# Windowed attention with two gated feed-forward layers: head units turned one slot later, zero products moved, first front product begun one step later

## Chip, cores and metric

One NeuronCore of a Trainium2 chip. The metric is the device time of one execution in microseconds (us), median of the runs of a kernel.

## What is computed

Attention of 2 batches x 8 heads, 768 positions, head size 64, with 4 sink keys and a window of 128; its output, as 1536 tokens of 512 features, goes through a SiLU-gated layer and a leaky-ReLU layer:

```python
scores = np.where(is_sink | in_window, scale * q @ k.T, -1e9)
a = exp(scores - max) / (sum + 1e-9);  attn = a @ v
x = attn.transpose(0, 2, 1, 3).reshape(1536, 512)
y = (silu(x @ w_gate) * (x @ w_val)) @ w_out          # d_ff 1536
h = y @ w_in2
out = (max(h, 0) + alpha * min(h, 0)) @ w_out2        # d_ff 2048
```

## The kernel before, in words

**Units and slots.** The attention is cut into 48 units: one tile of 128 queries for one pair of heads. One unit passes through seven steps on five engines: PE makes the scores (`scores`, L1833 to L1841), DVE masks them and takes the maximum (`take`, `maximum`), ACT takes exponentials and sums (`exps`), DVE inverts the sums (`invert`, L2286), POOL multiplies by the inverses (`normalise`, L1780), PE turns (transposes) the result (`turn`, L1861), DVE copies it out of PSUM under the window's triangles (`spread`, L2297), and PE multiplies by V (`values`, L1886; in the head with a product for the sinks, L1896). A list, `plan`, is written out ahead of time and every engine walks through it in order. Its item `slot` holds four unit numbers: scores of w; exponentials, inversion and normalising of w-1; turn of w-2; values of w-3 (`LAG = 3`).

**The head.** The first 16 units (`early`) are worked "pair by pair" with nothing else for PE to do: slots w = 0 to 18, which have indices 0 to 18. In a head slot PE does scores, then turn, then values. For units with sinks ACT copies the turned sink columns (`copy_sinks`, L2091) behind the exponentials of the slot; the product L1896 waits for that copy. The p tiles alternate between two PSUM halves, so scores of unit w wait for the exponentials of w-2. `keep_busy` (L2054) multiplies zeros, to keep PE occupied: 6 products at the start, 6 before scores of unit 2, and 2, 1, 1 and 2 before the turns of units 0, 1, 2 and 14. The first front product of the feed-forward layer ("begin") stands behind slot 16. In each head slot POOL also splits half a piece of weights into a high and a low part (`split_piece`, L1698 and L1699).

**The main part.** The other 32 units are spread over the products of the first layer ("front" and "back" chunks, L1932 and L2047), one slot every 4 us or so: w = 16 to 50, indices 19 to 53. There PE does scores, then values, then turn, then front or back products. POOL does, in this order, normalise of unit w-1 and then the jobs given to the slot (`in_slot`): two jobs in slots of even index, one in those of odd index, or one where sums (`tsum`) follow. A job is a whole piece of weights, or a sum. The pieces are numbered r in the order of the jobs; 0 to 5 are split in the head, 6 is the first of the main part. There are 4 buffers for raw pieces, so piece r can be loaded once piece r-4 has been split.

**The loads.** SP issues every load from one queue, in order, and waits on semaphores in between:

```python
for n in range(early, len(slot_plan) + 1):
    if n_pairs * c - 5 <= n and c < n_quads:
        load_values(c)      # waits: values of units < 4*(c-2)
        c += 1
    if n_pairs * c - 8 <= n and n % n_pairs == 0 and c < n_quads and c > RING + 1:
        load_keys(c)        # waits: scores of units < 4*(c-2)
    while r < len(raws) and slot_of_raw(r) <= n:
        load_piece(r)       # waits: piece r-4 split
        r += 1
```

`slot_of_raw(r)` is the index of the slot that holds the job that frees the buffer of piece r. So n counts slot indices, and the loads of keys and values (c is a group of four units) stand at fixed indices in the queue. Sorted by this loop the queue reads, before: v6, p10, k7, p11, p12, p13, p14, p15, v7, p16, k8, p17 and so on (k is keys and queries, v values, p a raw piece).

Of the kernel before, what the change touches and what calls it, by code (L numbers as in the profile page):

```python
# [804 lines left out]
def build_windowed(nc, qt, kt, vt, vs, pieces, alpha_t, out, n_batch, n_sink, ff_b, ff_c, scale):  # L805
# [7 lines left out]
    early = quads_t * n_pairs  # L813
# [61 lines left out]
    LAG = 3  # L875

    def slot(w, lo, hi):
        return ("slot", tuple(u if lo <= u < hi else None for u in range(w, w - LAG - 1, -1)))

    def fronts(g):  # L880

        return [("front", (g, f, part, half)) for part in range(parts[g[0]] - 1) for f in range(F) for half in range(2)]
# [24 lines left out]
    def emit_slot(item):  # L907
        plan.append(item)
        done = item[1][3]
        if done is not None and done % n_pairs == n_pairs - 1:  # L910
            c = done // n_pairs
            plan.append(("x", c))
            return [("x_rest", c)]
        return []
# [42 lines left out]
    first_g = groups_b[0]  # L957
    begun = {(first_g, 0, 0): n_k - 1}
    late_rest = []
    for w in range(early + LAG):  # L960
        item = slot(w, 0, early)
        rest = emit_slot(item)
        plan.extend(late_rest)
        late_rest = rest
        if w == early:
            plan.append(("begin", (first_g, 0, 0, 0)))
        if (item[1][3] or 0) == early - 1:
            plan.extend(rest)
# [161 lines left out]
    for what, key in chunks:  # L1130
        home = None
        if what == "back":
            g, t, d = key
            if g[0] == "B" and t != single:
                home = (rest_of_b if g != pair_b[-1] else (2, 3, 4, 0, 1, 2, 3, 4))[4 * (t - 1) + d]
            elif g[0] == "C" and (t != single or g[1] > 2):
                had["all"] = had.get("all", -1) + 1
                home = had["all"] % 3
            elif g == groups_c[2]:
                home = d % 2  # L1140
        elif what == "strip" or key[3] == 1 or (key[0][0] == "C" and key[0][1] > 2):
            continue
        if home is None:

            home = in_turn[(len(front_home) + len(back_home)) % 4]
# [143 lines left out]
    slot_plan = [n for n, (what, _) in enumerate(plan) if what == "slot"]  # L1289
    in_slot = [[] for _ in slot_plan]  # L1290

    def ready_at(job):
        what, key = job
        name = ("piece", key) if what == "piece" else ("sums", (key[0], key[1], key[2] // 2))
        return plan_at[cell_ahead[name]] if name in cell_ahead else -1

    next_job = first_pieces
    for n in range(early + LAG, len(slot_plan)):
        for _ in range(1 if n % 2 or plan[slot_plan[n] + 1][0] == "tsum" else 2):
            if next_job < len(jobs) and ready_at(jobs[next_job]) < slot_plan[n]:  # L1300
                in_slot[n].append(jobs[next_job])
                next_job += 1
# [3 lines left out]
    n = next(n for n, job in enumerate(late_jobs) if ready_at(job) >= turn_at)  # L1306
# [4 lines left out]
    with ctx:  # L1311
# [95 lines left out]
        att_ps = ctx.enter_context(nc.psum_tensor("att_ps", [P, 4 * BANK], F32))  # L1407
        ffn_ps = ctx.enter_context(nc.psum_tensor("ffn_ps", [P, 4 * BANK], F32))

        def bank(ps, n):  # L1410
            return ps[:, n * BANK:(n + 1) * BANK]

        def home(n, last):

            return ffn_ps if n < last and n % 2 else att_ps
# [10 lines left out]
        def before(n, last):  # L1426

            return n - 2 if n <= last else n - 1
# [115 lines left out]
        def head_sinks(u):  # L1544

            return u < early and has_prev(place(u)[0])

        def head_sinks_until(u):
            return sum(head_sinks(v) for v in range(u + 1))
# [103 lines left out]
        def _(pool):  # L1653
# [75 lines left out]
            def pair_sum(stage, n, m):  # L1729

                name = T_ORDER[stage][n]
                if stage == "B":
                    at = (slice(None), slice(None), block_cols(m))
                    if name == "T1":
                        pool.wait_ge(xcopy_done, 2 * m + 2)
                        pool.wait_ge(xlo_done, quads_t + 2 * m + 1)
                    elif name == "T2":
                        pool.wait_ge(xlo_done, quads_t + 2 * m + 2)
                else:
                    at = (slice(None), m, slice(None))  # L1740
                    if name == "T1":
                        pool.wait_ge(x2lo_done, x2_no[pair[0], m])
                        pool.wait_ge(evac_done, evac_no[pair_b[-1], pair[1], m])
                    elif name == "T2":
                        pool.wait_ge(evac_done, evac_no[pair_b[-1], pair[1], half_k + m])
                    elif name == "T4":
                        pool.wait_ge(x2lo_done, x2_no[pair[0], half_k + m])
                if n:
                    pool.wait_ge(tsum_done, tsum_no[stage, n - 1, m])
                q11, q21, q12, q22 = (q[at] for q in quarters[stage])  # L1750
                t1, t2 = (sum_sb(stage, T_ORDER[stage].index(t))[at] for t in ("T1", "T2"))
                a, b = {"T1": (q12, q11), "T2": (q22, t1), "T3": (q22, q12), "T4": (q21, t2)}[name]
                pool.tensor_tensor(sum_sb(stage, n)[at], a, b, ALU.subtract).then_inc(tsum_done, 1)
# [39 lines left out]
            n_slot = -1  # L1793
            for what, units in plan:
                if what == "tsum":
                    pair_sum(*units)
                if what != "slot":
                    continue
                n_slot += 1
                if units[1] is not None:  # L1800
                    normalise(units[1])
                if n_slot < early + LAG:
                    if n_slot in (early - 4, early - 3, early, early + 1):
                        split_v_sink(sinks_split // 2, sinks_split % 2)
                        sinks_split += 1
                    elif halves_split < 2 * first_pieces:
                        split_piece(jobs[halves_split // 2][1], 2, halves_split % 2)
                        halves_split += 1
                else:
                    for job in in_slot[n_slot]:  # L1810
                        do(job)
# [4 lines left out]
        def _(pe):  # L1816
# [24 lines left out]
                        last = pe.matmul(ps[:, 0:2 * cols], q, both, start=True, stop=True)  # L1841
                    last.then_inc(scores_done[h], 1)

            fills = {0: 2, 1: 1, 2: 1, early - 2: 2}

            def turn(u):
                s, n = divmod(u, n_pairs)
                if u == 0:
                    pe.wait_ge(pool_own, own["consts"])
                ahead = before(u, early)  # L1850
                if ahead >= 0:
                    pe.wait_ge(pt_done, ahead + 1)
                    if head_sinks(ahead):
                        pe.wait_ge(head_sink_done, head_sinks_until(ahead))
                    elif ahead % n_pairs == n_pairs - 1 and stacked_sinks(ahead // n_pairs):
                        pe.wait_ge(sink_done, sinks_until(ahead // n_pairs))
                if u in fills:
                    keep_busy(fills[u], bank(home(u, early), 2))
                pe.wait_ge(norm_done, u + 1)
                for h in range(2):  # L1860
                    last = pe.transpose(turn_ps(u)[:, block_cols(h)], p_sb[:, u % 8, h * (cols + n_sink):h * (cols + n_sink) + P], ident[:, :])  # L1861
                if head_sinks(u):
                    last = pe.transpose(turn_ps(u)[0:2 * n_sink, block_cols(2)], p_sb[:, u % 8, P:P + 2 * n_sink], ident[:, :])
                elif n == n_pairs - 1 and stacked_sinks(s):
                    pe.wait_ge(gathered, sinks_until(s))
                    last = pe.transpose(turn_ps(u)[0:stacked, block_cols(2)], p_sink[:, s % 2, :], ident[:, :])
                last.then_inc(turned, 1)
# [183 lines left out]
            def keep_busy(n, ps):  # L2051

                for _ in range(n):
                    pe.matmul(ps, h_hi[:, 0, 0:P], h_hi[:, 0, :], start=True, stop=True, skip_group_check=True)  # L2054
# [3 lines left out]
            for what, n in plan:  # L2058
                if what == "front":
                    front(*n)  # L2060
                elif what == "back":
                    back(*n)
                elif what == "strip":
                    strip(*n)
                elif what == "begin":
                    begin_front(*n)
                elif what == "slot":
                    if n[0] == 2:
                        keep_busy(6, bank(att_ps, 2))
                    if n[0] is not None:  # L2070
                        scores(n[0])
                    if n[2] is not None and n[2] < early:

                        turn(n[2])
                        if n[3] is not None:
                            values(n[3])
                    else:
                        if n[3] is not None:
                            values(n[3])
                        if n[2] is not None:  # L2080
                            turn(n[2])
# [452 lines left out]
```

## Time and profile before

| | us |
|---|---|
| median of 3 runs | 635.02 (634.78 to 650.35) |
| profiled execution, its own time | 635.71 |
| its span, first to last instruction | 634.0 |
| granted TensorE clock | 1.000 |

Times in the rows are microseconds from the start of the span; 1.7 us of the profiled execution lie around the span. "idle before" with a name is the time that the engine stood still ahead of an instruction, and what released it. PE's records overlap, since products are pipelined: the distance from start to start is what one costs.

### The profile page before, as it was taken

What the parts mean: (1) busy time and instruction counts of PE and PEld (TensorE: products, weight loads), DVE (VectorE), ACT (ScalarE), POOL (GpSimd) and SP (SyncE); (2) the same over time, 40 slices, a digit from 0 to 9 for tenths busy, and PEclk for the clock granted to TensorE, in tenths of its full rate; (3) what the DMA queues carried; (4) which work ended last, traced back from release to release, by engine and by line L of the source; (5) the groups of instructions that cost most, each with busy time, mean ns of one, the idle gap of its engine ahead of it and who ended that gap; (6) DMA issues with size and microseconds to landing.
All of it is one profiled execution on the core that took longest, in us unless ns stands there. A gap on an engine that the chain in (4) does not pass through costs nothing.

```text
span 634.0 us, 9482 instructions
## 1 busy us (share of the span) xinstructions
PE 624.4 (98%) x3113; PEld 488.7 (77%) x3113; DVE 410.7 (65%) x689; ACT 245.5 (39%) x597; POOL 452.7 (71%) x597
## 2 busy tenths in 40 slices
PE   8899999999999999999999999999999999999997
PEld 5557776777777888888887888887888888888886
DVE  4855476575476866565647474898686567756474
ACT  4646545536435542121212121445534324442150
POOL 6857778787788999998989664689999987810000
PEclk9999999999999999999999999999999999999999
DMA  9064333421213111121102322100222212000004
GB/s 309 19 189 146 98 104 117 134 68 52 66 68 100 34 34 39 66 87 42 68 34 66 98 70 66 33 18 18 67 67 67 68 66 84 18 0 1 0 18 182
DMA packets 34016, 45.69 MB, mean 72 GB/s; under 512 B 2888, under 2 KB 15176, under 8 KB 33968
## 3 DMA queue, kind: packets, MB, share of 16 engines
q1 hardware_dynamic: 33824, 44.83, 21.7%
q8 instruction: 25, 0.41, 0.3%
q10 hardware_dynamic: 144, 0.26, 0.2%
q14 instruction: 23, 0.19, 0.1%
HBM read 41.93 MB, written 3.15 MB: 71 GB/s over the span
## 4 chain that ended last, share of the span: by engine, by line
PE 93%; ACT 1%; DMA 1%; DVE 1%; POOL 1%; issue 1%; SPq 0%; DVEq 0%; ACTq 0%; POOLq 0%
PE ffn_ps L2047 29%; PE att_ps L2022 24%; PE ffn_ps L1932 14%; PE att_ps L2047 8%; PE ffn_ps L2022 7%; PE att_ps L1886 3%; PE att_ps L1841 3%; PE att_ps L1861 2%; PE att_ps L1932 1%; DMA raw_weights<-pieces 1%; POOL scratch L1780 1%; PE att_ps L1903 1%; DMA k_sb<-kt 1%; PE ffn_ps L1886 1%; ACT scratch L2104 1%
## 5 line engine op out<-in xcount | busy, mean ns | idle before, releaser
L1699 POOL TENSOR_TENSOR w_lo<-raw_weights,w_hi 128x512 fp32r<-128x512 f32 (+1 forms) x128 | 155.4, 1214 | 10.3
L1698 POOL CAST w_hi<-raw_weights 128x512 fp32r<-128x512 f32 (+1 forms) x128 | 80.9, 632 | 33.5 <-PE ffn_ps L2047 17.2
L2409 DVE TENSOR_TENSOR scratch<-ffn_ps,scratch 128x512 f32<-128x512 f32 x108 | 74.1, 687 | 34.8 <-PE ffn_ps L2047 34.2
L1727 POOL TENSOR_TENSOR w_lo<-part_sum,w_hi 128x256 fp32r<-128x256 f32 x80 | 59.7, 747 | 6.4
L1932 PE MATMUL ffn_ps<-x_hi,w_hi 128*128 128x512 f32 x152 | 61.9, 407 | 0.1
L1932 PE MATMUL ffn_ps<-x_hi,w_lo 128*128 128x512 f32 x152 | 59.4, 391 | 0.0
L1932 PE MATMUL ffn_ps<-x_lo,w_hi 128*128 128x512 f32 x152 | 59.3, 390 | 0.0
L1780 POOL TENSOR_TENSOR scratch<-scratch,inv 128x264 f32<-128x264 f32 (+1 forms) x48 | 30.4, 634 | 31.5 <-DVE inv L2286 31.3
L2047 PE MATMUL ffn_ps<-h_hi,w_hi 128*128 128x512 f32 x130 | 51.6, 397 | 0.0
L2047 PE MATMUL ffn_ps<-h_hi,w_lo 128*128 128x512 f32 x130 | 50.7, 390 | 0.0
L2047 PE MATMUL ffn_ps<-h_lo,w_hi 128*128 128x512 f32 x130 | 50.6, 389 | 0.0
L2193 ACT ACTIVATE value_sb<-att_ps 128x512 f32<-128x512 f32 x14 | 8.4, 599 | 94.2 <-PE att_ps L2022 94.2
L2022 PE MATMUL att_ps<-t_hi,w_hi 128*128 128x512 f32 x112 | 44.2, 394 | 0.0
L2022 PE MATMUL att_ps<-t_hi,w_lo 128*128 128x512 f32 x112 | 44.0, 393 | 0.0
L2022 PE MATMUL att_ps<-t_lo,w_hi 128*128 128x512 f32 x112 | 43.7, 390 | 0.0
L2022 PE MATMUL att_ps<-x_hi,w_hi 128*128 128x512 f32 x108 | 42.8, 396 | 0.0
L2022 PE MATMUL att_ps<-x_hi,w_lo 128*128 128x512 f32 x108 | 42.4, 393 | 0.0
L2022 PE MATMUL att_ps<-x_lo,w_hi 128*128 128x512 f32 x108 | 42.1, 390 | 0.0
L2269 DVE COPY_PREDICATED att_ps<-take_prev,att_ps 128x256 f32<-128x256 int32 x36 | 15.3, 426 | 39.5 <-PE att_ps L1841 28.7
L1726 POOL CAST w_hi<-part_sum 128x256 fp32r<-128x256 f32 x80 | 35.8, 447 | 5.1
L2097 ACT ACTIVATE bias<-top 128x2 f32<-128x2 f32 x48 | 9.7, 202 | 72.0 <-DVE top L2281 72.0
L2182 ACT ACTIVATE gate_sb<-gate_sb,minus_alpha 128x512 f32<-128x512 f32 x48 | 34.8, 725 | 1.6
(213 smaller groups left out, 1586.0 us busy)
## 6 DMA issues: line engine op xcount, KB each, us to landing
raw_weights<-pieces SPq DMA_DIRECT2D x122, 256.0 KB, 2.7
k_sb<-kt SPq DMA_DIRECT2D x12, 264.0 KB, 3.5
v_sb<-vt SPq DMA_DIRECT2D x12, 256.0 KB, 3.6
out<-scratch SPq DMA_DIRECT2D x12, 256.0 KB, 2.0
q_sb<-qt SPq DMA_DIRECT2D x11, 256.0 KB, 4.2
scratch<-vs SPq DMA_DIRECT2D x1, 384.0 KB, 7.0
q_sb<-qt ACTq DMA_DIRECT2D x1, 256.0 KB, 3.5
scratch<-vs SPq DMA_DIRECT2D x1, 16.0 KB
```

Of the source, the lines that this page charges most:

```text
L1698: chain(pool.tensor_copy(hi, raw[:, r % n_raw, at]))
L1699: last = pool.tensor_tensor(lo, raw[:, r % n_raw, at], hi.bitcast(F32), ALU.subtract)
L1726: chain(pool.tensor_copy(hi, s))
L1727: pool.tensor_tensor(lo, s, hi.bitcast(F32), ALU.subtract).then_inc(split_done, 1)
L1780: pool.tensor_tensor(rows, rows, inv[:, u % 4, :].unsqueeze(2).to_broadcast([P, 2, cols - at]), ALU.mult).then_inc(norm_done, 1)
L1841: last = pe.matmul(ps[:, 0:2 * cols], q, both, start=True, stop=True)
L1886: last = pe.matmul(x[d, :], v_sb[:, g, ring, d], pt_sb[:, u % 2, m, h, :], start=n == 0 and m == 0, stop=not has_prev(c), skip_group_check ...
L1932: last = pe.matmul(ps, w_parts[a][:, block_cols(kk)], x_parts(kk)[b], start=kk == 0 and (a, b) == (0, 0), stop=kk == n_k - 1 and (a, b) == ...
L2022: last = pe.matmul(ps, w_parts[a][:, block_cols(at * half_k + kk)], b_parts[b][:, kk, :], start=first and kk == 0 and (a, b) == (0, 0), st ...
L2047: last = pe.matmul(ps, lhs, rhs, start=f == 0 and (a, b) == (0, 0), stop=f == F - 1 and (a, b) == (1, 0))
L2182: act.activation(gate_of(h), gate_of(h), ACT.Copy, scale=minus_alpha[:, col:col + 1]).then_inc(relu_done, 1)
L2409: ins = dve.tensor_tensor(to, back_ps(key), total, ALU.add)
```

## The change

Head slots hold other units: scores of w, exponentials to normalising of w-1, turn of w-3 (was w-2), values of w-4 (was w-3). So the head has 20 slots, w = 0 to 19. "begin" stands behind slot 18, which holds the turn of unit 15; before it stood behind the slot with the turn of unit 14. The zero products are now 6 before scores of unit 2 and 4 before scores of unit 3, beside the 6 at the start; those before the turns are gone. The start of POOL's jobs and the end of its head work go by the new length. SP's loop is not touched.

```diff
+    HEAD_LAG = 4
+
+    def head_slot(w):
+
+        return ("slot", tuple(u if 0 <= u < early else None for u in (w, w - 1, w - HEAD_LAG + 1, w - HEAD_LAG)))
...
-    for w in range(early + LAG):
-        item = slot(w, 0, early)
+    for w in range(early + HEAD_LAG):
+        item = head_slot(w)
         rest = emit_slot(item)
         plan.extend(late_rest)
         late_rest = rest
-        if w == early:
+        if w == early + 2:
             plan.append(("begin", (first_g, 0, 0, 0)))
...
     next_job = first_pieces
-    for n in range(early + LAG, len(slot_plan)):
+    for n in range(early + HEAD_LAG, len(slot_plan)):
         for _ in range(1 if n % 2 or plan[slot_plan[n] + 1][0] == "tsum" else 2):
...
-                if n_slot < early + LAG:
+                if n_slot < early + HEAD_LAG:
                     if n_slot in (early - 4, early - 3, early, early + 1):
...
-            fills = {0: 2, 1: 1, 2: 1, early - 2: 2}
+            fills = {2: 6, 3: 4}
...
-                if u in fills:
-                    keep_busy(fills[u], bank(home(u, early), 2))
                 pe.wait_ge(norm_done, u + 1)
...
                 elif what == "slot":
-                    if n[0] == 2:
-                        keep_busy(6, bank(att_ps, 2))
+                    if n[0] in fills:
+                        keep_busy(fills[n[0]], bank(att_ps, 2))
```

## Rows read from the trace of the kernel before

**Rows 1.** The page: busy time of PE, share of the span, instructions.

```profile
PE 624.4 (98%) x3113; PEld 488.7 (77%) x3113; DVE 410.7 (65%) x689; ACT 245.5 (39%) x597; POOL 452.7 (71%) x597
```

**Rows 2.** Waits of the whole span: in total, times, longest.

```profile
POOL w_hi L1698 <- DMA raw_weights<-pieces: 8.5, 6, 3.0
...
PE ffn_ps L1861 <- POOL scratch L1780: 3.4, 6, 0.8
```

**Rows 3.** Busy time by engine in head slots 8 to 11.

```profile
20.75:29.39 8.64, 7.47 (x70) 4.20 (x68) 6.99 (x19) 5.57 (x29) 6.88 (x13) 1.00 0.01 4
```

**Rows 4.** Timeline of PE in the head: start, duration, instruction, idle before.

```profile
1.52 2.93 PE L2054 MATMUL att_ps<-h_hi 128*128 128x512 f32 x6 [1.52 <-DVE h_hi L2441]
4.51 1.25 PE L1841 MATMUL att_ps<-k_sb,q_sb 64*128 64x264 f32 x4
...
22.83 0.72 PE L1841 MATMUL ffn_ps<-k_sb,q_sb 64*128 64x264 f32 x4
24.02 0.41 PE L1861 MATMUL ffn_ps<-ident,scratch 128*128 128x128 f32 x2 [0.48 <-POOL scratch L1780]
...
25.31 0.72 PE L1841 MATMUL att_ps<-k_sb,q_sb 64*128 64x264 f32 x4
...
35.44 0.49 PE L1833 MATMUL ffn_ps<-k_sb,q_sb 64*128 64x128 f32 x4
...
42.09 0.44 PE L1886 MATMUL ffn_ps<-scratch,v_sb 128*64 128x128 f32 x4
```

**Rows 5.** Timeline of ACT in head slot 15: the copy of sink columns.

```profile
38.85 0.25 ACT L2091 ACTIVATE scratch<-ffn_ps 8x128 f32<-8x128 f32 x1
```

**Rows 6.** Timeline of SP's queue: the issues of keys 7 to 11.

```profile
55.76 0.55 SPq L1598 DMA_DIRECT2D k_sb<-kt  x1
...
75.10 0.55 SPq L1598 DMA_DIRECT2D k_sb<-kt  x1
...
93.58 0.55 SPq L1598 DMA_DIRECT2D k_sb<-kt  x1
...
112.26 0.56 SPq L1598 DMA_DIRECT2D k_sb<-kt  x1
...
131.93 0.56 SPq L1598 DMA_DIRECT2D k_sb<-kt  x1
```

**Rows 7.** Timeline of POOL: pieces that waited for their load, and the normalising behind them.

```profile
60.78 0.61 POOL L1698 CAST w_hi<-raw_weights 128x512 fp32r<-128x512 f32 x1 [0.94 <-DMA raw_weights<-pieces]
...
62.72 1.07 POOL L1780 TENSOR_TENSOR scratch<-scratch,inv 128x264 f32<-128x264 f32 x1
...
118.92 0.61 POOL L1698 CAST w_hi<-raw_weights 128x512 fp32r<-128x512 f32 x1 [2.98 <-DMA raw_weights<-pieces]
...
120.84 0.63 POOL L1780 TENSOR_TENSOR scratch<-scratch,inv 128x264 f32<-128x264 f32 x1
```

**Rows 8.** Timeline of PE, main part: scores of unit 19 (54.91), turn of 18 (60.50), and so on.

```profile
54.91 0.50 PE L1835 MATMUL att_ps<-k_sb,q_sb 64*128 64x132 f32 x4 [0.43 <-ACT scratch L2104]
...
60.50 0.44 PE L1861 MATMUL att_ps<-ident,scratch 128*128 128x128 f32 x2
...
74.28 0.72 PE L1841 MATMUL att_ps<-k_sb,q_sb 64*128 64x264 f32 x4
...
79.64 0.44 PE L1861 MATMUL att_ps<-ident,scratch 128*128 128x128 f32 x2
...
92.97 0.49 PE L1833 MATMUL att_ps<-k_sb,q_sb 64*128 64x128 f32 x4
...
98.67 0.44 PE L1861 MATMUL att_ps<-ident,scratch 128*128 128x128 f32 x2
...
121.62 0.41 PE L1861 MATMUL att_ps<-ident,scratch 128*128 128x128 f32 x2 [0.19 <-POOL scratch L1780]
...
131.07 0.50 PE L1835 MATMUL att_ps<-k_sb,q_sb 64*128 64x132 f32 x4
...
136.67 0.44 PE L1861 MATMUL att_ps<-ident,scratch 128*128 128x128 f32 x2
```

## The prediction

> **What bounds the kernel now.** The page first: PE is busy for 624.4 of 634.0 us [rows 1]. So only 9.6 us of the span are free of PE work, and a change can win little but lose as much as it likes: every wait that it puts in front of PE is added to the end. Next the list of waits by engine: PE waited 3.4 us in six pieces for POOL's normalising, and all six stand in the head [rows 2]. The table of stretches shows a group of four head slots: 8.64 us long, PE busy for 7.47, and DVE and POOL at 6.99 and 6.88, not far behind [rows 3]. The timeline of PE shows where it comes from: scores of unit 9 start at 22.83, the turn in the same slot only at 24.02, after 0.48 us of idle [rows 4]. Outside the head PE hardly waits, and so what the head gains reaches the end, if nothing behind it gets worse. That was my second reading: POOL waited 8.5 us in six pieces for loads of weights [rows 2]. Today this costs PE 0.19 us, once [rows 8], since it ends just in time. The change moves POOL's jobs and leaves SP's queue where it is, so I followed that queue item by item.
>
> **The head, gain.** With the turn at w-3 the normalised unit is a whole slot older when PE comes to it. In a group of four slots it is done 1.3 us or more ahead (normalising 0.6 us, slots of about 1.9), so the 3.4 us of waits go. Of the zero products, six go and four come (two before the turn of 14 are a further 0.5 us on the path; those before turns 0 to 2 and the four new ones stand where PE waits for exponentials of the first units, and cost about nothing). That is 3.9 us at most.
>
> What is late next is ACT's copy of the sink columns. It stands last in ACT's slot, behind the exponentials: in slot 15 scores start at 35.44 and the copy ends at 38.85 + 0.25 = 39.10, 3.66 us later [rows 4, 5]. The product of the next slot needs it, before and after the change alike, but the slots get shorter. Slots with tile 0 cost PE about 1.2 us and the next ones 2.1, together 3.3, where the copy with the product behind it asks for 3.6: 0.3 us three times, 0.9. After slot 15 PE arrives 2.6 us behind the scores (1.5 for the slot, 0.45 for a turn, 0.6 for values) at a copy that ends 3.7 behind them: 1.1 us. Gain of the head: 3.9 - 0.9 - 1.1 = **1.9, taken as 2.0 us**; bounds 0.5 (DVE and POOL, near full, delay more) and 3.9. The first front product moved behind the last turn is the same product at another place in the order: it is work that covers the wait for the values of unit 15, which end at 42.5 today [rows 4], and I cost it at nothing (if the cover is missing, 0.3 us).
>
> **The main part, loss.** The head has one more slot, so each slot of the main part has an index higher by one. POOL's first job moves with it (index 20), but the choice of two jobs for even indices now falls on the other slots of w, and SP's loads of keys and values stand at the old indices, one slot early in w. SP's queue then reads v6, k7, p10, p11, p12, p13, p14, v7, p15, k8, p16 instead of v6, p10, k7, p11 and so on: one piece fewer ahead of each barrier. What the barrier waits for is unchanged: keys 7 wait for the scores of unit 19, keys 8 for those of 23, keys 9 of 27, keys 11 of 35. POOL needs more by then: in the slot w=18 it has pieces 9 and 10 to split, and behind them in its queue stands the normalising of unit 18, which PE turns in slot w=20. But piece 10 is now behind keys 7, and they go out only with the scores of unit 19. So POOL stands still over a whole slot, and behind it the normalising, and behind that PE's turn with all front products.
>
> The price follows from rows that show the same chain one slot later. Scores of 19 at 54.91, keys 7 issued at 55.76 (0.85 later) [rows 6, 8]; the piece behind them lands and POOL starts at 60.78 (5.02 later) [rows 7]; the piece takes 62.72 - 60.78 = 1.94; normalising to turn takes 121.62 - 120.84 = 0.78 [rows 7, 8]. Together 8.59 us behind the scores of 19. PE wants the turn of 18 at 60.50, 5.59 behind them [rows 8]. **Stall 3.0 us.** The same at the other barriers, with scores, issue and turn from [rows 6, 8]:
> - keys 8, piece 16, turn of 22: 0.82 + 5.02 + 1.94 + 0.78 = 8.56, wanted at 79.64 - 74.28 = 5.36: 3.2 us.
> - keys 9, piece 22, turn of 26: 8.35, wanted at 98.67 - 92.97 = 5.70: 2.65 us.
> - keys 10: the sums behind slots 27 and 28 take a job away from each, and the two orders meet again; piece 28 waits for its load (2.98 us) and the turn of 31 for 0.19, as now. No change.
> - keys 11, piece 33 (now the second job of w=34), turn of 34: 8.60, wanted at 136.67 - 131.07 = 5.60: 3.0 us.
>
> Sum 3.0 + 3.2 + 2.65 + 3.0 = **11.9 us**. The barrier of keys 10 shows that the load can take 6.66 instead of 5.02 (112.26 to 118.92) [rows 6, 7]; with that at all four the sum is 11.9 + 4 x 1.64 = 18.5. I take 5.02, since it stands at keys 7 itself and the queue behind keys 11 is short. Behind slot 34 the jobs are sums, which need no load, and further on pieces are far ahead of their users: nothing more. Values 7 and on hold back one piece as well (15, 21), but that one lands before the piece behind the keys and so ends inside the same stall.
>
> Sum: 635.7 (the profiled execution, whose span is 634.0) - 2.0 + 11.9 = 645.6; the median of the runs is 0.7 lower, so **644.9 us**, 1.6% slower.
>
> **The clock.** TensorE's granted clock is 1.00 in the stretch of the head that I read [rows 3]. But six zero products at the start take 2.93 us and four scores at 4.51 take 1.25, against 0.72 for four of the same form at 22.83 [rows 4]: the engine runs at 1.2 GHz for its first 4 us of work and at 2.4 after them. That stretch cost some 2 us. So if a stall of 3 us throws it back to the low level, each costs 2 us more. No idle stretch of that length after the start is in this trace. The Trainium skill (TensorE: Matmul & The Clock Gate, Why this matters for your kernels) asks for no long idle gaps between bursts of products, or the clock halves; by it each stall forecast here would be priced as in the rival of the falling clock below. What it says of keeping the engine busy at the start speaks against taking zero products out of the first slots too.
>
> **Rivals.**
> - *The queue doesn't bite*, since a load lands sooner than I think or POOL's order leaves room: only the head's gain, 635.0 - 2.0 = 633.0 (631 to 634.5). For it: POOL had 0.9 to 3 us of such waits already and PE paid 0.19. Against: 8.6 against 5.6 us is a clear gap; even a load that lands 2 us sooner leaves a stall of 1 us. Chance 0.14.
> - *It bites in part*, with one or two of the four stalls hidden: 636 to 641. Chance 0.09.
> - *The clock falls* in the stalls: four times 2 us more, 652.9, slower by more than 2%; it decides at a stall of 3 us between the units, and from two falls on the time is past 648. Chance 0.12.
> - *Loads take 6.66 us* at most barriers, with many pieces queued behind one another: 644.9 + up to 6.6, 648 to 651.5. Chance 0.13.
> - The forecast, 641 to 648: chance 0.52.
>
> **Range and chances.** A measurement of this kernel tells about 2% from no change, 12.7 us. Leaving out the first rival below and a tail above, the range is 636 to 653. Slower by over 2% is past 647.7: 0.12 + 0.13 + 0.01 = 0.26. Faster by over 2% would need more than all of PE's idle time: 0.01. Within: 0.73.
>
> **What the profile after would show.** PE's waits for L1780 in the head gone, and groups of four head slots at 7.4 to 7.9 us; waits of PE's turn (L1861) for POOL's normalising of 2.6 to 3.3 us each, at about 58, 81, 103 and 144 us, some 12 us in total; POOL's idle time before L1698 up from 8.5 to over 20 us with the load as releaser; in SP's queue keys 7 ahead of any piece. PE's product of the front at one spacing on both sides of a stall, if the clock holds. Wrong would be: head waits that move to ACT's copy by more than 2 us, or waits of PE that are missing in the main part, which would mean that the loads are not what holds POOL.

## Result and the profile after

The changed kernel takes **656.10 us** (median of 4 runs, 655.83 to 657.79), the kernel before 635.03 (median of 4): a ratio of **1.0339 [1.0317, 1.036]**, 3.4% slower. The forecast was 644.9 with a range to 653, so the time lies 3.1 us above the range. A run of the kernel before that took 650.35 us, and others like it, are left out of every ratio here, though a median takes in all runs unless it says otherwise. The profiled execution took 656.12 us, its span is 654.4 (634.0 before), the granted clock 0.984 (1.000 before).

The page of the changed kernel: busy time of PE, then its busy share and its granted clock in 40 slices of 16.4 us each. Against [rows 1] PE is busy for 8.4 us more, though it does two instructions fewer.

```profile
PE 632.8 (97%) x3111; PEld 494.6 (76%) x3111; DVE 405.0 (62%) x689; ACT 246.2 (38%) x597; POOL 451.3 (69%) x597
...
PE   8997977998999999999999999999999999999998
PEclk9998989997999999999999999999999999999999
```

In the busy row PE is below 90% in slices 1, 4, 6, 7, 10 and 40 (a 9 stands for 90% or more), and the granted clock is below 90% in slices 4, 6 and 10. The kernel before has an 8 in slices 1 and 2 and a 7 in slice 40, 9 in all others, and nothing but 9 in its clock. So there are two losses in the same part of the kernel: time in which PE stands still, and time in which it works at a lower clock. The second sits inside "busy", and the list of waits doesn't show it.

Waits of the changed kernel, whole span (lines are shifted by 4 to 6: L1704 is L1698 of before, L1786 is L1780, L1865 is L1861), to be put beside [rows 2]:

```profile
POOL w_hi L1704 <- DMA raw_weights<-pieces: 35.8, 12, 6.4
...
PE att_ps L1865 <- POOL scratch L1786: 14.2, 4, 4.1
```

The 3.4 us of PE's waits in the head are gone. In their place stand four waits of 14.2 us together, and POOL's waits for loads have gone from 8.5 to 35.8 us. The timeline of PE shows the four, and the head ahead of them:

```profile
19.01 0.72 PE L1847 MATMUL att_ps<-k_sb,q_sb 64*128 64x264 f32 x4
...
26.98 0.72 PE L1847 MATMUL att_ps<-k_sb,q_sb 64*128 64x264 f32 x4
...
35.75 0.66 PE L1890 MATMUL ffn_ps<-scratch,v_sb 128*64 128x128 f32 x8 [0.51 <-DVE scratch L2301]
...
42.49 0.50 PE L1841 MATMUL att_ps<-k_sb,q_sb 64*128 64x132 f32 x4
...
53.35 0.50 PE L1841 MATMUL att_ps<-k_sb,q_sb 64*128 64x132 f32 x4 [0.43 <-ACT scratch L2108]
...
62.65 0.66 PE L1865 MATMUL att_ps<-ident,scratch 128*128 128x128 f32 x2 [3.64 <-POOL scratch L1786]
62.96 0.78 PE L1936 MATMUL ffn_ps<-x_hi,w_hi 128*128 128x512 f32 x1
...
68.17 0.40 PE L1936 MATMUL ffn_ps<-x_hi,w_hi 128*128 128x512 f32 x1
68.40 0.40 PE L1936 MATMUL ffn_ps<-x_lo,w_hi 128*128 128x512 f32 x1
...
88.51 0.62 PE L1865 MATMUL att_ps<-ident,scratch 128*128 128x128 f32 x2 [4.12 <-POOL scratch L1786]
...
112.30 0.52 PE L1865 MATMUL att_ps<-ident,scratch 128*128 128x128 f32 x2 [3.38 <-POOL scratch L1786]
...
154.71 0.66 PE L1865 MATMUL att_ps<-ident,scratch 128*128 128x128 f32 x2 [3.01 <-POOL scratch L1786]
```

Scores of unit 19 start at 53.35, the turn of unit 18 at 62.65 instead of some 3.6 us sooner. Behind it 12 products take 68.17 - 62.96 = 5.21 us from start to start, 0.43 each; then they go on at 0.23. What holds the turn is seen in SP's queue, beside [rows 6]:

```profile
43.76 0.58 SPq L1611 DMA_DIRECT2D v_sb<-vt  x1
54.20 0.54 SPq L1604 DMA_DIRECT2D k_sb<-kt  x1
...
55.47 6.81 SPq L1616 DMA_DIRECT2D raw_weights<-pieces  x5
```

and in POOL's timeline, beside [rows 7]:

```profile
59.97 0.61 POOL L1704 CAST w_hi<-raw_weights 128x512 fp32r<-128x512 f32 x1 [6.43 <-DMA raw_weights<-pieces]
...
61.88 0.63 POOL L1786 TENSOR_TENSOR scratch<-scratch,inv 128x264 f32<-128x264 f32 x1
...
85.83 0.61 POOL L1704 CAST w_hi<-raw_weights 128x512 fp32r<-128x512 f32 x1 [4.55 <-DMA raw_weights<-pieces]
...
109.63 0.61 POOL L1704 CAST w_hi<-raw_weights 128x512 fp32r<-128x512 f32 x1 [3.67 <-DMA raw_weights<-pieces]
...
152.03 0.61 POOL L1704 CAST w_hi<-raw_weights 128x512 fp32r<-128x512 f32 x1 [3.49 <-DMA raw_weights<-pieces]
```

Read as one chain: no piece is issued between values 6 (43.76) and keys 7 (54.20, 0.85 behind the scores that they wait for); the first piece behind the keys lets POOL start at 59.97; POOL takes 1.91 for it; the normalising at 61.88 is followed 0.77 later by PE's turn. It is the chain of the prediction, link by link.

**Where the 20.4 us of span went.** The scores of unit 16 start at 42.49; before they started at 44.05, so the head gives 1.56 back. The stalls add 3.64 + 4.12 + 3.38 + 3.01 = 14.15, and the 0.19 of before [rows 8] is gone: +13.96. What is left is 20.4 + 1.56 - 13.96 = **8.0 us**, to which no wait belongs. The table of stretches shows what it is (columns: stretch, its length, busy time and instructions of PE, PEld, DVE, ACT, POOL, then the granted clock, DMA share, GB/s):

```profile
60.00:64.00 4.00, 1.35 (x5) 1.19 (x6) 0.65 (x2) 0.81 (x5) 3.84 (x5) 0.66 0.50 155
64.00:66.00 2.00, 2.00 (x6) 1.62 (x5) 0.96 (x2) 0.00 (x0) 1.94 (x4) 0.50 0.03 12
66.00:68.00 2.00, 2.00 (x6) 1.52 (x6) 0.00 (x0) 0.00 (x0) 1.92 (x3) 0.50 0.00 0
68.00:70.00 2.00, 2.00 (x12) 1.38 (x10) 0.00 (x0) 0.00 (x0) 1.55 (x2) 0.98 0.00 0
...
90.00:92.00 2.00, 2.00 (x6) 1.52 (x6) 1.69 (x3) 0.00 (x0) 1.94 (x4) 0.51 0.00 0
...
114.00:116.00 2.00, 2.00 (x7) 1.57 (x6) 1.13 (x2) 0.00 (x0) 1.92 (x4) 0.53 0.00 0
...
156.00:158.00 2.00, 2.00 (x6) 1.59 (x5) 0.10 (x1) 0.00 (x0) 1.92 (x4) 0.50 0.00 0
```

From 64 to 68 PE is busy all the time and does 6 instructions in 2 us where it does 12 from 68 on: the clock is at 0.50, the level of 1.2 GHz. It came down in the stall and is back at 68. The last three rows show the same behind the other three stalls. A full PE row with a low instruction count beside it is the sign to look for.

The distances of the products give the price a second time. Behind the first stall it is 12 x (0.43 - 0.23) = 2.4 us. Behind the others PE's timeline has 7, 8 and 11 products at 0.43 before they go on at 0.23, some 1.5, 1.6 and 2.3 us more, and together 7.8 (an estimate from these distances).

### The profile page after: what moved, and what is told of

Its sections match the earlier page's. It is cut to its first block, busy times and chain, and to the rows that moved or that the text cites. A ratio compares the mean times of both kernels' runs of the same rounds, so it can differ in the third digit from the quotient of the medians.

```text
span 654.4 us, 9479 instructions
## 1 busy us (share of the span) xinstructions
PE 632.8 (97%) x3111; PEld 494.6 (76%) x3111; DVE 405.0 (62%) x689; ACT 246.2 (38%) x597; POOL 451.3 (69%) x597
## 4 chain that ended last, share of the span: by engine, by line
PE 89%; DMA 5%; POOL 2%; ACT 2%; DVE 1%; issue 1%; SPq 0%; DVEq 0%; POOLq 0%; ACTq 0%
PE ffn_ps L2051 27%; PE att_ps L2026 23%; PE ffn_ps L1936 14%; PE att_ps L2051 7%; PE ffn_ps L2026 6%; DMA raw_weights<-pieces 4%; PE att_ps L1890 3%; PE att_ps L1847 2%; PE att_ps L1865 2%; POOL w_lo L1705 1%; PE att_ps L1936 1%; ACT scratch L2108 1%; POOL w_hi L1704 1%; DMA k_sb<-kt 1%; PE ffn_ps L1847 0%
## 5 line engine op out<-in xcount | busy, mean ns | idle before, releaser
L1704 POOL CAST w_hi<-raw_weights 128x512 fp32r<-128x512 f32 (+1 forms) x128 | 78.9, 617 | 62.0 <-DMA raw_weights<-pieces 35.8
L1936 PE MATMUL ffn_ps<-x_hi,w_hi 128*128 128x512 f32 x152 | 64.5, 424 | 0.1
L1936 PE MATMUL ffn_ps<-x_hi,w_lo 128*128 128x512 f32 x152 | 61.7, 406 | 0.0
L1936 PE MATMUL ffn_ps<-x_lo,w_hi 128*128 128x512 f32 x152 | 61.6, 406 | 0.0
L1786 POOL TENSOR_TENSOR scratch<-scratch,inv 128x264 f32<-128x264 f32 (+1 forms) x48 | 30.7, 639 | 26.2 <-DVE inv L2290 26.0
L2186 ACT ACTIVATE gate_sb<-gate_sb,minus_alpha 128x512 f32<-128x512 f32 x48 | 34.8, 725 | 1.6
```

Source lines behind the costliest of these rows:

```text
L1704: chain(pool.tensor_copy(hi, raw[:, r % n_raw, at]))
L1786: pool.tensor_tensor(rows, rows, inv[:, u % 4, :].unsqueeze(2).to_broadcast([P, 2, cols - at]), ALU.mult).then_inc(norm_done, 1)
L1936: last = pe.matmul(ps, w_parts[a][:, block_cols(kk)], x_parts(kk)[b], start=kk == 0 and (a, b) == (0, 0), stop=kk == n_k - 1 and (a, b) == ...
L2186: act.activation(gate_of(h), gate_of(h), ACT.Copy, scale=minus_alpha[:, col:col + 1]).then_inc(relu_done, 1)
```

## Experiments

The theory after the result: SP's loads of keys and values stand one slot too early against POOL's jobs, PE stalls four times for that, and each stall lowers the clock behind it. The rivals: the new head itself costs the time; the choice of two jobs in even slots does; the 8 us are something other than the clock. "Before" is always the kernel before, run on the same chip beside the experiment. The changed kernel itself was not run again beside them; it has 656.10 against 635.03 for the kernel before, which took 635.45 to 635.53 beside the experiments.

### The queue moved along by one slot

In the changed kernel SP's two conditions take n - 1, so that keys and values stand in the same slots of w as before. The jobs stay as the change has them.

```diff
-                if n_pairs * c - 5 <= n and c < n_quads:
+                if n_pairs * c - 5 <= n - 1 and c < n_quads:
...
-                if n_pairs * c - 8 <= n and n % n_pairs == 0 and c < n_quads and c > RING + 1:
+                if n_pairs * c - 8 <= n - 1 and (n - 1) % n_pairs == 0 and c < n_quads and c > RING + 1:
```

> The changed kernel with one edit: SP's conditions for keys and values count from the longer head (n - 1 in place of n). Theory (the stalls come from keys and values that stand one slot too early in SP's queue): the pieces 10, 16, 22 and 33 are again ahead of their barrier, the four waits of PE for the normalising (14.2 us) go, with them the stretches at half clock; only the head's gain is left: 633.5 us, 22.6 less than the changed kernel. Rival (the order of the jobs, two in other slots, holds POOL by itself): waits of PE of several us stay, 640 to 656. Rival (the head itself costs): waits gone and the time still over 636.

Measured: 633.52 us (633.10 to 633.59), before 635.45, ratio 0.9967 [0.9955, 0.998]. SP's queue of this kernel now has two pieces between values 6 and keys 7:

```profile
44.13 0.58 SPq L1611 DMA_DIRECT2D v_sb<-vt  x1
44.76 1.80 SPq L1616 DMA_DIRECT2D raw_weights<-pieces  x2
54.56 0.55 SPq L1604 DMA_DIRECT2D k_sb<-kt  x1
```

Its waits: POOL waits 9.9 us for loads in place of 35.8, near to [rows 2], and PE's turn waits for the normalising 0.2 us in place of 14.2.

```profile
POOL w_hi L1704 <- DMA raw_weights<-pieces: 9.9, 7, 2.3
```

So two conditions in a queue that the change did not touch are worth 656.10 - 633.52 = 22.6 us, and what is left of the change is a gain of a third of a per cent. The whole loss hangs on the numbering.

### The queue and the jobs moved along

The same, and the choice of one or two jobs goes by n - 1 too.

```diff
-        for _ in range(1 if n % 2 or plan[slot_plan[n] + 1][0] == "tsum" else 2):
+        for _ in range(1 if (n - 1) % 2 or plan[slot_plan[n] + 1][0] == "tsum" else 2):
```

> The changed kernel with SP's conditions and the choice of slots with two jobs both counted from the longer head, so that the main part is that of before, in the order of its units. Theory: 633.4 us, waits of PE for normalising in the main part 0.2 us in all as before; the difference to before, 1.6 us, is the head alone. Rival (the head's gain is lost again on the way): 635.

Measured: 633.30 us (632.90 to 634.50), ratio 0.9968 [0.9958, 0.9978]. It can't be told from the kernel above; with the queue right, no cost shows for the place of the second job. In its trace no turn in the main part waits for the normalising.

### Only the jobs moved along

The last edit alone, SP's queue as in the change.

> The changed kernel with one edit: the slots that get two jobs are again those of before in the order of the units (n - 1 in place of n); SP's queue stays as the change left it. Theory (the stall needs both, a load one slot too early in the queue and a second job ahead of the normalising): with one job in the slots w=18, 22 and 26 the normalising gets through, the stalls of 3 to 4 us go; where a slot with two jobs now meets late loads (w=31, and the sums behind piece 33) 0.5 to 2 us each may stay: 634 to 637 us, clock 1.00. Rival (the queue alone makes the loss): 650 to 656.

Measured: 644.69 us (640.51 to 647.04), before 635.53, ratio 1.0132 [1.0098, 1.0166]. This missed: it is 7.7 us above the upper end expected. I had followed keys only. Its timelines show the stalls at the barriers of values (a barrier is a load in the queue that waits, with everything behind it). The first of them, SP:

```profile
69.17 0.55 SPq L1611 DMA_DIRECT2D v_sb<-vt  x1
69.76 1.20 SPq L1616 DMA_DIRECT2D raw_weights<-pieces  x2
```

POOL and PE, whose turn waits behind it:

```profile
73.04 0.61 POOL L1704 CAST w_hi<-raw_weights 128x512 fp32r<-128x512 f32 x1 [3.99 <-DMA raw_weights<-pieces]
...
74.95 0.62 POOL L1786 TENSOR_TENSOR scratch<-scratch,inv 128x264 f32<-128x264 f32 x1
```

```profile
75.72 0.41 PE L1865 MATMUL att_ps<-ident,scratch 128*128 128x128 f32 x2 [1.83 <-POOL scratch L1786]
```

The piece for the second job of slot w=21 is freed one slot later than in the change and so falls behind values 7, which wait for the values of unit 19. PE waits four times, 7.3 us in all and at most 2.3 at a time. In the profiled run (640.51) the clock held at 1.000; the other three had 0.992 to 0.995 and took 644.3 to 647.0. So the jobs alone take off half of the loss and do not heal the change; a queue one slot too early costs with either choice of jobs, through values with one and through keys with the other.

### The old head with the queue one slot too early

The kernel before, its head, zero products and "begin" untouched; SP's conditions and the choice of jobs take n + 1 instead of n (and SP's loop starts one index sooner). This is the loss of the change without any other part of it.

```diff
-        for _ in range(1 if n % 2 or plan[slot_plan[n] + 1][0] == "tsum" else 2):
+        for _ in range(1 if (n + 1) % 2 or plan[slot_plan[n] + 1][0] == "tsum" else 2):
...
-            for n in range(early, len(slot_plan) + 1):
-                if n_pairs * c - 5 <= n and c < n_quads:
+            for n in range(early - 1, len(slot_plan) + 1):
+                if n_pairs * c - 5 <= n + 1 and c < n_quads:
...
-                if n_pairs * c - 8 <= n and n % n_pairs == 0 and c < n_quads and c > RING + 1:
+                if n_pairs * c - 8 <= n + 1 and (n + 1) % n_pairs == 0 and c < n_quads and c > RING + 1:
```

> The kernel before, its head untouched, with only the indices of the main part taken one higher for SP's keys and values and for the slots with two jobs. Theory: this alone makes the loss: 635.0 + 14.0 of stalls + 8 of half clock = 657 us, four waits of PE for the normalising of units 18, 22, 26 and 34. Rival (the stalls need the new head, for example since SP's first loads come earlier): 635 to 645.

Measured: 657.60 us as the median of three runs (654.87 to 657.93; a fourth, of 670.96 at a clock of 0.957, is left out), ratio 1.0336 [1.0312, 1.0359]. Its waits show those of the old head (3.2, as in [rows 2]) and the stalls of the changed kernel side by side (14.9 in five pieces, of which 14.2 in four lie between 58 and 160 us):

```profile
PE att_ps L1861 <- POOL scratch L1780: 14.9, 5, 4.2
...
PE ffn_ps L1861 <- POOL scratch L1780: 3.2, 6, 0.8
```

The new head is not where the loss comes from.

### The stalls filled with products

In the changed kernel PE does 13 products of 512 columns with real data ahead of the turns of units 18, 22, 26 and 34. They write into the bank that the turn then overwrites, so the result is unchanged. 13 x 0.23 = 3.0 us is nearly the stall: the stall stays, but PE isn't idle in it.

```diff
+                if u in (18, 22, 26, 34):
+                    for _ in range(13):
+                        pe.matmul(bank(att_ps, 2), x_hi[:, 0, 0:P], x_hi[:, 0, :], start=True, stop=True, skip_group_check=True)
                 pe.wait_ge(norm_done, u + 1)
```

> The changed kernel with 13 products of real data, written to the bank of the turn and overwritten by it, ahead of PE's wait for the normalising of units 18, 22, 26 and 34. They take 13 x 0.23 = 3.0 us, inside the stalls of 3.0 to 4.1. Theory (the stalls themselves cost 14 us and a fall of the granted clock behind them 8 us): the stalls stay as gaps of 1 us or less beside the products, the clock stays at 2.4 GHz, 648 us. Rival (the rest of the loss has another cause than the clock): 656.

Measured: 647.46 us (647.10 to 648.37), ratio 1.0193 [1.0178, 1.0209], granted clock 1.000 in all four runs. Its timeline of PE at the first stall:

```profile
58.90 3.26 PE L1865 MATMUL att_ps<-x_hi 128*128 128x512 f32 x13
62.48 0.44 PE L1868 MATMUL att_ps<-ident,scratch 128*128 128x128 f32 x2 [0.31 <-POOL scratch L1786]
62.67 0.48 PE L1939 MATMUL ffn_ps<-x_hi,w_hi 128*128 128x512 f32 x1
...
65.49 0.39 PE L1939 MATMUL ffn_ps<-x_hi,w_hi 128*128 128x512 f32 x1
```

The turn comes at 62.48 (62.65 in the changed kernel): the same stall. The 12 products behind it take 65.49 - 62.67 = 2.82 us instead of 5.21, so 2.4 us of clock at this stall. POOL's wait for loads is unchanged, 34.8 in 12 pieces. The kernel does more work and is 656.10 - 647.46 = **8.6 us faster** (by the two ratios, 1.0339 and 1.0193, it would be 9.3); that is the price of the clock, and it is near the 8.0 us left over above.

### The stalls half filled

The same with 6 products, which leaves 1.6 to 2.6 us of idle time at each.

> The changed kernel with 6 products of real data instead of 13 ahead of the four awaited turns. They cover 1.4 us of each stall and leave gaps of 1.6 to 2.5 us. Theory (only the long gaps let the clock fall): clock 1.00 and the time of the run with 13 products, 647.5, since the stalls end by the load and not by PE. Rival (gaps of 2 us are enough): a part of the 8 us comes back, 650 to 655.

Measured: 650.99 us, ratio 1.0253 [1.0205, 1.0301], but from 648.18 to 657.52 over four runs, with clocks of 0.997, 0.989, 0.997 and 0.995. Two of the four stalls in the profiled run, in PE's timeline:

```profile
84.68 0.69 PE L1868 MATMUL att_ps<-ident,scratch 128*128 128x128 f32 x2 [2.09 <-POOL scratch L1786]
...
150.71 0.44 PE L1868 MATMUL att_ps<-ident,scratch 128*128 128x128 f32 x2 [2.63 <-POOL scratch L1786]
```

and the stretches around them:

```profile
80.00:88.00 8.00, 5.91 (x27) 4.43 (x28) 4.28 (x9) 1.85 (x7) 5.68 (x8) 0.79 0.44 157
...
150.00:158.00 8.00, 7.29 (x41) 5.52 (x42) 2.79 (x7) 2.22 (x7) 7.49 (x14) 1.00 0.00 0
```

The clock fell behind an idle time of 2.09 us and did not behind those of 1.6, 2.06 and 2.63. So the expectation, a clock of 1.00 and 647.5, missed. At this length the outcome differs from place to place, and the mean clock from run to run; the length of the gap alone doesn't decide it. What does is left open. The clock isn't the whole spread either: 0.997 against 0.989 of some 650 us is about 5 us (an estimate), and the two runs lie 657.52 - 648.18 = 9.3 us apart.

### The zero products alone

The kernel before with 6 zero products before scores of unit 2 and 4 before those of unit 3, and none before turns. Those of unit 3 write to the other half of PSUM than in the changed kernel.

```diff
-            fills = {0: 2, 1: 1, 2: 1, early - 2: 2}
+            fills = {2: 6, 3: 4}
...
-                if u in fills:
-                    keep_busy(fills[u], bank(home(u, early), 2))
...
-                    if n[0] == 2:
-                        keep_busy(6, bank(att_ps, 2))
+                    if n[0] in fills:
+                        keep_busy(fills[n[0]], bank(att_ps if n[0] == 2 else ffn_ps, 2))
```

> The kernel before with only its zero products changed as in the change (none before the turns, 4 before scores of unit 3, these in the other half of PSUM), units turned as before. Theory (zero products stand where PE waits anyway): 635.0, within 0.5 of before. Rival (they are a part of the gain): 633.5 to 634.3; rival (they keep the clock up in the first slots): slower by 1 us or more, a clock under 1.00.

Measured: 635.04 us over 12 runs, before 635.53 (19 runs), ratio 0.999 [0.9978, 1.0002]: no difference that can be told, though the interval leaves room for a gain of up to 1.4 us (0.22% of 635). Nine runs took 634.34 to 636.47 at a clock of 1.000, three took 647.40 to 649.55 at 0.968 to 0.973. No trace of one of the three was kept.

### The first front product at its old place

The kernel with queue and jobs moved along, with "begin" behind slot 16 again.

```diff
-        if w == early + 2:
+        if w == early:
```

(The edits of the queue and the jobs are as above.)

> The kernel with SP's conditions and the jobs counted from the longer head, but the first front product begun behind slot 16 as before the change, in place of behind the last turn. Theory (the product is the same work at another place): 633.3 as with it, within 0.3. Rival (behind the last turn it covers the wait for the values of unit 15): slower by 0.4 to 0.7 us, 633.9.

Measured: 633.38 us against 633.30, ratio 0.9962 [0.9948, 0.9977]. The place of "begin" is worth nothing that can be told, as forecast. What is left for the gain of 2 us is the later turn, with whatever the zero products give: at most 1.4 us by the interval above, and in the trace of that run the scores of unit 16 start at 43.55 in place of 44.05. The later turn was not run without them, so how the gain is split is not shown.

### Without the four zero products before unit 3

The kernel with queue and jobs moved along, with `fills = {2: 6}`.

> The kernel with SP's conditions and the jobs counted from the longer head, without the 4 zero products before scores of unit 3. They take 0.9 us in the profile of the changed kernel, ahead of scores that are ready at about 9.1 us there. Theory: up to 0.4 us less, 632.9 to 633.3, clock 1.00 all through. Rival (they keep the clock up in the sparse first slots): a granted clock under 1.00 in the first 20 us and 634 to 636.

Measured: median 633.57 us, ratio 0.998 [0.9957, 1.0003], but the 12 runs fall into two groups: eight from 632.62 to 633.78 at a clock of at least 0.999, four at 637.48, 640.23, 640.24 and 643.81 at 0.979 to 0.989. The profiled run is one of the four. Its stretches in the head:

```profile
12.00:16.00 4.00, 2.91 (x21) 1.71 (x23) 3.40 (x9) 3.01 (x17) 3.83 (x7) 0.80 1.05 313
16.00:20.00 4.00, 4.00 (x21) 2.19 (x23) 1.52 (x4) 2.13 (x12) 2.95 (x6) 0.50 0.23 82
20.00:24.00 4.00, 4.00 (x24) 2.15 (x21) 1.38 (x5) 1.22 (x6) 1.70 (x3) 0.50 0.00 0
24.00:30.00 6.00, 6.00 (x40) 3.12 (x39) 4.23 (x12) 3.29 (x15) 3.37 (x6) 0.66 0.02 4
```

Two of these stretches in the kernel with the four products:

```profile
12.00:16.00 4.00, 3.76 (x36) 2.21 (x37) 3.76 (x10) 3.02 (x16) 2.50 (x5) 1.00 1.06 290
...
20.00:24.00 4.00, 3.60 (x34) 2.04 (x34) 3.23 (x9) 3.05 (x14) 3.84 (x8) 1.00 0.02 6
```

In the first, PE stands still for 1.44 us ahead of the scores at 13.09; then the clock falls to 0.50 and stays there for over 8 us, though PE is busy all the time. But the two runs differ before the first of the four products would have come. The six zero products before scores of unit 2, which both kernels have, in the run without the four and then in the run with them:

```profile
6.71 2.93 PE L2058 MATMUL att_ps<-h_hi 128*128 128x512 f32 x6
```

```profile
6.65 1.64 PE L2058 MATMUL att_ps<-h_hi 128*128 128x512 f32 x6
```

So the slow products of the start lasted longer in the run without the four (its scores at 9.57 still took 1.25 us), and what is missing behind them can't be the reason for that part. (The granted clock is given as 1.00 for these first microseconds in both; the lower level is read from the durations.) The other eight runs of the same kernel kept a clock of at least 0.999 without the four products.

The rival on record, that the four keep the clock up, was priced at 634 to 636; four runs of 12 went that way and took 4 to 11 us more than the other eight. None of the 27 runs of the four kernels that have the new head with all zero products and a queue in time had a clock below 0.999, which speaks for the four products as a guard. Against it, the old head with all ten products (the run with the zero products alone) had three of 12 runs at 0.968 to 0.973. That the four products prevent the fall is therefore suggested and not shown; when nothing falls, leaving them out gains nothing that can be told.

### The queue two slots later still

The changed kernel with the jobs moved along and SP's conditions at n - 3, and so with more pieces ahead of each barrier than the kernel before has.

> The kernel with the jobs counted from the longer head and SP's conditions two slots later still (n - 3), so that more pieces stand ahead of each barrier of keys and values. Theory: POOL's waits for loads in the main part (5 us and more in the kernel with n - 1) shrink to 1 us or less, the waits of PE for the normalising (0.2 to 0.9 us) go: 632.5 to 633.2. Rival (keys or values then come late for PE): waits of PE for loads, over 634.

Measured: 633.34 us (633.14 to 635.11), before 635.48, ratio 0.9967 [0.9954, 0.998]. POOL waits for loads 6.3 us in 4 pieces (12.8 in 7 with the queue and the jobs moved along by one). The expectation was 1 us or less and 632.5 to 633.2, so the waits missed and the time lies 0.1 above. Half of POOL's waits went and the time stayed the same as with n - 1 (633.30): what POOL still waits for is hidden.

## Why the prediction was wrong

**The mechanism held.** SP's queue one slot too early, four stalls of the turn behind the normalising behind a piece behind the keys: forecast to begin at about 58, 81, 103 and 144 us, the waits began at 59.01, 84.39, 108.92 and 151.70 (the starts of the turns, 62.65, 88.51, 112.30 and 154.71, less the idle time before them). Each is later than forecast because the earlier ones, and the clock, push it back. The old head with a wrong queue (657.60) and the new head with a right one (633.52) show that the loss needs nothing else. Keys 10 stayed harmless, as forecast.

**The step that failed: the clock.** The prediction priced it rightly and put it in the wrong place. Its rival "the clock falls", four times 2 us, chance 0.12, is what happened: 8.0 us by the sum of the span, 8.6 by the filled stalls, 7.8 by the distances of the products. The forecast took none of it, with the remark that no idle stretch of that length after the start is in the trace. That was a reason to leave it unknown, not to count it as nothing: at the start, behind 1.52 us in which the engine had done nothing, four scores took 1.25 us against 0.72 later [rows 4]. The Trainium skill (TensorE: Matmul & The Clock Gate, Why this matters for your kernels) asks for no long idle gaps between bursts of products, or the clock halves; by that rule the forecast would have been 652.9, and the trace agrees: four of four gaps of 3.0 to 4.1 us were followed by products at 0.43 us instead of 0.23. In the half-filled stalls one gap of 2.09 us was followed by a fall too.

**A term of the wrong size: the load.** From the issue of the keys to POOL's start I took 5.02 us. Measured were 59.97 - 54.20 = 5.77, then 6.05 (79.78 to 85.83), 5.59 (104.04 to 109.63) and 5.14 (146.89 to 152.03), between the value taken and the bound of 6.66. The stalls came to 14.15 instead of 11.85, 2.3 us more. The other links fit: the issue 0.85 behind the scores, 1.91 for the piece (1.94), 0.77 from normalising to turn (0.78).

**The head** gave 1.6 us instead of 2.0. The group of four slots of units 8 to 11 takes 26.98 - 19.01 = 7.97 us, just above the forecast of 7.4 to 7.9 (8.64 in [rows 3]). The waits for L1780 are gone in this trace; in that of the kernel with queue and jobs moved along, which has the same head, 0.89 and 0.40 us of them are left. The wait of 1.1 us for ACT's copy behind slot 15 did not come; a wait of 0.51 for DVE's spread stands there instead (35.75). With the queue mended the median is 635.45 - 633.30 = 2.15 us better. The traces with this head put the scores of unit 16 anywhere from 42.14 to 43.45 (44.05 before), so what the head gives back differs from execution to execution, 0.6 to 1.9 us.

**The sum of the error**: 656.1 - 644.9 = 11.2 is 8.0 of clock (a term that the forecast's sum put at nothing), 2.3 of stalls, 0.4 of head and 0.7 that the median was taken to lie below the profiled execution and didn't, less the 0.19 of [rows 8]. Clock and load were priced as rivals one at a time, though both can come together; that is how each lay inside the range and the time outside it.

## What to carry to other kernels

Where a list of work is renumbered, go through every queue that counts in its indices: here two conditions that the diff does not touch cost 22.6 us and hid a gain of 2.1. When a forecast puts new idle time of about 3 us in front of TensorE, put the clock behind it into the sum and not among the rivals, and read a stretch for the instruction count and the granted clock beside the busy time. And rivals that don't exclude each other must be added up for the range.

## What the runs showed of the hardware

- **A gap costs more than its length.** Idle gaps of 3.0 to 4.1 us ahead of dense products lowered the granted clock to 0.50 four times in four; it cost 2.4 us at the first and 8.0 / 4 = 2.0 on the mean. Of four gaps of 1.6 to 2.6 us in one traced run only that of 2.09 did so, not the one of 2.63, and four runs of that kernel took from 648 to 658 us.
- **The low level can last.** In the main part, with products of 512 columns behind the turn, the clock was back 3.7 to 5.7 us after the turn (62.65 to 68.17, and 88.51 to 92.18). In the head, with small products, one traced run stayed at 0.50 for over 8 us with PE busy throughout (16 to 24 us, without the four zero products). Why the one is long and the other short was not tried.
- **The granted clock of the rows is not the whole clock.** In the first 6 us it is given as 1.00 while four scores take 1.25 us against 0.72 later [rows 4].
- **A load behind keys and queries** took 5.1 to 6.1 us from the issue of the keys until POOL could start on the piece.
